# The second block's slope joined as h + (1-a) relu(-h), with h read from PSUM

## The reference

```python
X = np.fft.fft(np.fft.fft(x, axis=1), axis=2).real
h = X @ w_in                                    # block 1
g = np.where(h > 0.0, h, np.exp(np.minimum(h, 0.0)) - 1.0)
x = g @ w_out
h = x @ w_in                                    # block 2
g = np.maximum(h, 0.0) + alpha * np.minimum(h, 0.0)   # one alpha in 0 .. 0.3 per hidden unit
out = g @ w_out
```

## Time and profile before

| | value |
|---|---|
| median of 3 runs | 1039.86 us (1038.32 to 1041.12) |
| span of the profiled execution | 1040.5 us |
| busy TensorE, ScalarE, VectorE | 98%, 65%, 63% of the span |
| granted TensorE clock, mean | 0.997 |
| block 2 | from about 514 us to the end |

### The profile page before, as it was taken

One profiled execution on the slowest core, in us unless ns is written; L12 is line 12 of the kernel. 1 busy time (PEld: TensorE's weight loads), 2 busy tenths in 40 slices (PEclk: granted clock), 3 DMA queues, 4 the chain that ended last, 5 costly groups with the idle time before them and its releaser, 6 DMA issues.

```text
span 1040.5 us, 13229 instructions
## 1 busy us (share of the span) xinstructions
PE 1018.8 (98%) x4858; PEld 861.7 (83%) x4858; DVE 652.1 (63%) x676; ACT 673.9 (65%) x769; POOL 112.6 (11%) x101
## 2 busy tenths in 40 slices
PE   6799899999999999999999999999999999999998
PEld 6799788888888888888888888888888888888886
DVE  4344888988889888888855544544545454544444
ACT  3343787888888878887866556556655656555553
POOL 3693121212120210000000000000000000000000
PEclk9899999999999999999999999999999999999999
DMA  8637300302102002011020010002002001000101
GB/s 226 164 125 267 106 21 11 111 10 67 54 20 101 10 0 91 0 41 41 1 77 0 1 63 18 0 0 81 0 0 81 0 0 43 34 1 1 41 1 42
DMA packets 17358, 50.64 MB, mean 49 GB/s; under 512 B 1520, under 2 KB 10032, under 8 KB 14640
## 3 DMA queue, kind: packets, MB, share of 16 engines
q1 hardware_dynamic: 14208, 40.70, 11.7%
q0 software_dynamic: 3120, 9.54, 3.1%
HBM read 29.92 MB, written 20.32 MB: 48 GB/s over the span
## 4 chain that ended last, share of the span: by engine, by line
PE 95%; DMA 2%; DVE 2%; ACT 1%; issue 0%; SPq 0%; DVEq 0%; ACTq 0%
PE ACC L447 16%; PE ACC L448 16%; PE ACC L452 16%; PE PQ L431 8%; PE PQ L430 8%; PE PQ L429 8%; PE PQ L323 2%; PE PQ L400 2%; PE PQ L401 2%; PE PQ L406 2%; PE PQ L402 2%; PE PQ L405 2%; PE PQ L407 2%; PE PQ L404 2%; DMA xr<-in_x 2%; PE PQ L352 1%
## 5 line engine op out<-in xcount | busy, mean ns | idle before, releaser
L447 PE MATMUL ACC<-Gh,W 128*128 128x512 f32 (+1 forms) x768 | 297.1, 387 | 1.8 <-DVE eo_st L705 1.0
L448 PE MATMUL ACC<-Gl,W 128*128 128x512 f32 (+1 forms) x768 | 296.2, 386 | 0.0
L743 DVE TENSOR_TENSOR Gl<-G,Gh 128x1024 fp32r<-128x1024 f32 (+1 forms) x96 | 115.4, 1203 | 212.5 <-ACT Gh L562 212.5
L452 PE MATMUL ACC<-Gh,W 128*128 128x512 f32 (+1 forms) x768 | 233.9, 386 | 0.0
L641 ACT ACTIVATE H<-PQ 128x1024 f32<-128x1024 f32 (+1 forms) x96 | 97.1, 1011 | 130.4 <-PE PQ L431 130.4
L447 PEld LDWEIGHTS ACC<-Gh,W 128*128 128x128 f32 x768 | 144.1, 188 | 34.6 <-issue 2.7
L448 PEld LDWEIGHTS ACC<-Gl,W 128*128 128x128 f32 x768 | 144.3, 188 | 28.2
L452 PEld LDWEIGHTS ACC<-Gh,W 128*128 128x128 f32 x768 | 143.4, 188 | 25.1
L562 ACT ACTIVATE Gh<-G 128x1024 fp32r<-128x1024 f32 (+1 forms) x96 | 100.1, 1042 | 74.1 <-PE ACC L452 70.4
L430 PE MATMUL PQ<-y_hl,W 128*128 (+2 forms) x384 | 148.0, 385 | 0.0
L431 PE MATMUL PQ<-y_hl,W 128*128 (+2 forms) x384 | 148.0, 385 | 0.0
(11 more groups left out here) (78 smaller groups left out, 1148.8 us busy)
## 6 DMA issues: line engine op xcount, KB each, us to landing
eo_scratch<-eo_st SPq DMA_DIRECT2D x12, 640.0 KB, 3.9
EO<-eo_scratch SPq DMA_DIRECT2D x6, 1280.0 KB, 7.9
xr<-in_x SPq DMA_DIRECT2D x16, 384.0 KB, 6.9
raw<-in_w POOLq DMA_DIRECT2D x24, 256.0 KB, 3.2
y_scratch<-y_st SPq DMA_DIRECT2D x5, 1024.0 KB, 4.8
y_in<-y_scratch SPq DMA_DIRECT2D x5, 1024.0 KB, 6.9
out_y<-y_st SPq DMA_DIRECT2D x5, 1024.0 KB, 4.8
stage<-in_w1a POOLq DMA_DIRECT2D x4, 256.0 KB, 5.5
```

Of the source, the lines that this page charges most:

```text
L447: mm(o, W[:, 0, sl], Gh[:, j, c:c + w], start=f == 0, stop=False)
L448: mm(o, W[:, 0, sl], Gl[:, j, c:c + w], start=False, stop=False)
L452: ins = mm(o, W[:, 1, sl], Gh[:, j, c:c + w], start=False, stop=f == NF - 1)
L743: tt(Gl[:, j, 0:n], G[:, j, 0:n], f32(Gh[:, j, 0:n]), ALU.subtract).then_inc(lo_ready, 1)
```

## The change

The join computes G = (1 - alpha) relu(-h) + h, which for h > 0 is h and for h < 0 is h - (1 - alpha) h = alpha h. So H = relu(h) is no longer needed in block 2: ScalarE's pass at L641 and the wait ahead of it go, the join's third operand is PQ in PSUM instead of H in SBUF, and the small tensor of 16 scalars per partition holds 1 - alpha instead of -alpha. Since VectorE now reads PQ, `up2` waits for `g_ready`, which the join raises, instead of `act_ready`, which ScalarE's pass L643 raises. Block 1 is not touched.

```diff
-    nalpha = at("nalpha", 36 * KB + 4 * NF, [PT, NF], fp32)
+    slope = at("slope", 36 * KB + 4 * NF, [PT, NF], fp32)
@@ gpsimd, once
-            chain(gp.tensor_scalar(nalpha[:, :], alpha_sb[:, :], -1.0, 0.0, ALU.mult, ALU.add))
+            chain(gp.tensor_scalar(slope[:, :], alpha_sb[:, :], -1.0, 1.0, ALU.mult, ALU.add))
@@ up2
                 if isinstance(t, int) and s < 2:
                     pe.wait_ge(comb_ready, S1 + s - 1)
                 else:
-                    pe.wait_ge(act_ready, S1 + s - 1)
+                    pe.wait_ge(g_ready, S1 + s - 1)
@@ scalar, second
                 act.wait_ge(up_done, s + 1)
-                act.wait_ge(g_ready, s - 1)
-                fn(H[:, f % 2, 0:n], PQ[:, f % 2, 0:n], ACT.Relu)
                 act.wait_ge(lo_ready, s - 1)
                 fn(G[:, f % 2, 0:n], PQ[:, f % 2, 0:n], ACT.Relu, scale=-1.0).then_inc(act_ready, 1)
@@ vector, prelu
-                stt(G[:, j, 0:n], G[:, j, 0:n], nalpha[:, f:f + 1], H[:, j, 0:n], ALU.mult, ALU.add).then_inc(g_ready, 1)
+                stt(G[:, j, 0:n], G[:, j, 0:n], slope[:, f:f + 1], PQ[:, j, 0:n], ALU.mult, ALU.add).then_inc(g_ready, 1)
```

## The result

The changed kernel takes 1047.47 us (median of 4 runs, 1047.18 to 1049.34), the kernel before 1039.72 us in the same comparison: a ratio of 1.0079, 95% interval 1.0065 to 1.0093. It is 7.75 us slower; forecast were 7.1. The profiled execution took 1049.34 us, with a span of 1047.5, so 1.84 us lie outside the span.

A forecast was written before the change was run, and what follows sets the result against it. TensorE's stream without a hole bounds block 2. Lateness 5.46 us, nine restarts 1.53 and the tenth place 0.11 give 7.1, added to 1039.86: 1047.0 us, own range 1044.9 to 1049.3, with run scatter 1043.6 to 1050.2.

The forecast's parts named there:

- What bounds the kernel: Block 2: TensorE busy 87.00 of 87.00 us, so any new wait of TensorE lengthens the kernel by its full amount.
- The saved pass: Block 2, ScalarE's L641: 96 passes of 1.01 us, 97.1 us removed beside matmuls; gain taken as nothing.
- The new wait, slice by slice: Block 2: up(s+2) waits for the end of join(s); lateness against up's old start sums to 5.46 us.
- 84 pairs: Block 2: of 94 pairs of join(s) and up(s+2), 84 have slack of 0.86 us or more.
- The sign of being right: At up2's first line, f = 8 and 11 of tiles 0 to 4: ten matmul waits, nine of 0.4 to 0.8 us.
- The join's price: VectorE's join reading PSUM stays at 1.28 us, as from SBUF, with 0.05 us either way for the bounds.
- The restart: TensorE after each stall: 0.06 us to start plus 0.11 to get going, 0.17; nine stalls 1.53 us, tenth place 0.11.
- the ten places: Tiles 0 to 4, after f = 6 and 9, where the next tile's split precedes the join: nine late, one 0.06 us early.
- The sum: Block 2's ten places: 5.46 lateness + 1.53 restarts + 0.11 tenth place = 7.1 us, bounds 5.0 to 9.4.
- earlier split: Rival: ScalarE's y pass, then split, Gl and join come earlier, so no wait; no change, 1039.9 us; chance 0.10.
- faster matmuls: Rival: 97 us less ScalarE traffic lets block 2's matmuls run closer together; faster, 1037 us; chance 0.04.
- fall of the clock: Rival: TensorE's granted clock falls after a stall, making stalls longer; 1052 to 1100 us; chance 0.05.

The follow-up runs named there:

- the two kernels that keep the change and lose the waits: Changed kernel with ScalarE's y pass ahead of Gh: 1041.01 us, ratio 0.9999; changed kernel with VectorE's low half of the split one slice later: 1040.09 us, ratio 0.9989.
- the first four experiments: Kernel before with only the new wait, 1048.08 us; changed kernel with y pass ahead of Gh, 1041.01; split later at both places, 1040.09; at first only, 1043.38.
- the doubled operation: VectorE's low half of the split computed twice at the ten places: 1059.14 us in the changed kernel, 1040.01 us in the kernel before.

## Why the prediction was right

- **What bounds the kernel.** TensorE's stream had no hole in block 2, and every added wait showed up in the time. The saved pass gave nothing: the two kernels that keep the change and lose the waits have ratios of 0.9999 and 0.9989, and their block 2 differs from that of before by 0.05 us. Two readings about ScalarE were off, and neither enters the sum. The idle time in front of its pass over h (130.4 us) did not grow; the one in front of Gh did, from 70.4 to 146.4 us. And its busy time fell by 87 us, not by 97: the two passes over h lasted 1.01 us but started 0.92 us apart, so they overlapped in the trace, and busy time counts the overlap once.
- **The new wait, slice by slice.** The places, their number and their sizes were all in the trace of before: ends of joins against starts of up. 84 pairs were called free, and the difference of starts grows at none of them, but for the restart just behind a stall. The sign of being right, ten waits of a matmul with nine of 0.4 to 0.8 us, came out as nine waits of 0.30 to 0.61 us and ten waits of weight loads: the idle time before a matmul is counted from the modelled end of the one before it, and is shorter than the delay of its start.
- **The join's price.** Taken as unchanged, measured 4 ns shorter. The bound of 0.05 us either way was wide enough.
- **The restart.** Taken as 0.17 us for each stall, from one row. Over the ten places (7.33 - 5.46 + 0.06) / 10 is 0.19 us. The missing 0.02 us is the pace behind the stall: in the timeline above the next matmuls follow each other by 0.23 to 0.24 us (557.50, 557.74, 557.97), while the free stream goes at 5.44 / 24 = 0.227.
- **The sum.** 7.1 us forecast, 7.33 by the starts of up, 7.0 by the two spans, 7.75 by the medians. The spans differ by 0.3 us less because block 2 starts 0.32 us earlier in the changed kernel's execution. The rest is the scatter of single executions: the 31 runs of the kernel before that belong to the first four experiments lie between 1037.64 and 1046.00 us.
- **What was put loosely.** The prediction set a span of 1040.5 us beside a median of whole runs and called the profile 0.64 us above it. In the changed kernel's profiled execution 1.84 us lie outside the span; if as much does in the kernel before, that execution took 1042.3 us. The sum was a difference and is untouched.
- **The rivals.** No earlier split: it starts at the same distance from TensorE. No faster matmuls: 386 in 87 us at most, as before. No fall of the clock: granted 1.00 in every window read. On the clock the Trainium skill (TensorE: Matmul & The Clock Gate, the part on oscillation) warns of idle gaps; gaps of up to 1.6 us, as with the doubled operation in the changed kernel (mean granted clock 1.000), did not bring it on here.

## What to carry to other kernels

When a change hands a buffer back from another engine than before, line up two columns of the old trace: when the new last reader finishes and when the writer comes back. Each place where the reader finishes after the writer is back is a stall that the old kernel does not show, and it should be looked for above all where other work has been slipped into the reader's queue. Here 96 passes removed from an engine with slack were worth nothing, while the order of work in two engines' queues was worth 0.7% as soon as the bounding engine waited for it.

## Hardware, as the runs showed it

- A TensorE stream of matmuls of 512 columns, stopped by a semaphore, lost about 0.19 us on top of the wait (mean of the ten places): 0.05 us from the releasing engine's end, 0.34 instead of 0.23 us to the next matmul, and a slightly slower pace for some matmuls.
- VectorE's operation with two tensors and a scalar per partition took 1275 ns with one tensor in PSUM and 1279 with both in SBUF (1024 columns of 4 bytes).
- In the loops over tiles VectorE's split starts 0.34 us after ScalarE's y pass ends (552.17 + 1.04 = 553.21 against 553.55); in the unrolled tile 4 of the kernel before it was 0.04 (900.64 + 1.04 against 901.72). In the loop VectorE's queue runs two register operations of the split's line in between (from 553.25 to 553.50); in tile 4 the trace shows none. Leaving them out wasn't tried.
